# Outputs of the recurrence leave TensorE transposed, with state and values as stationary operands

## The chip, the cores and the metric

The program runs on one core of one Trainium2 chip. The metric is the device time of one execution in microseconds, lower is better. Times of the kernel before are given as the median of three runs; one further execution was recorded by the profiler, and every duration below comes from that one.

## The reference, cut to what matters

Three stages follow each other: a recurrence with one 48x48 state per batch and head (4 batches, 8 heads, 768 time steps), a gated network over 3072 tokens of width 384, and a mixture of eight experts. The change touches the first stage and its hand-over to the second.

```python
B, H, S, D = q.shape                       # 4, 8, 768, 48
k_n = k / (norm(k) + 1e-06)
for t in range(S):
    y[:, :, t] = einsum('bhd,bhde->bhe', q[:, :, t], state)
    v_old = einsum('bhde,bhd->bhe', state, kt)
    state = state + bt * einsum('bhd,bhe->bhde', kt, vt - v_old)
x = y.transpose(0, 2, 1, 3).reshape(B * S, H * D)
gate = 1 / (1 + exp(-(x @ w_gate)))
x = (gate * (x @ w_val)) @ w_out           # then: argmax expert, relu(x @ w1) @ w2, times the gate weight
```

## The kernel before

The program is written by hand, engine by engine, with semaphores; the order in each engine's text is the order in which it works. There is no scheduler.

**Recurrence.** The 768 steps of each batch are cut into chunks of 128 tokens, so there are NG = 24 groups of 128 tokens by 8 heads, worked through batch by batch, chunk after chunk. Two heads make a pair: NPAIR = 4. Inside a group the recurrence becomes a triangular system. A blocked inversion in LEVELS = 7 levels solves it: on each level TensorE forms masked products (L989), VectorE masks them (`level_mask`, L549), TensorE multiplies twice (L997, L1000) and ScalarE copies back (L776, L778). Group g is inverted in step s = g. Group cg = s - 1 is finished in the same step from the inverse found one step earlier: `keys_state` (L956), values W (L1027), `outputs_y` (L1033, L1035), `state_update` (L1043), `y_transposes` (L1049).

**Gated network.** It works on macro tiles of two groups (TB = 256 tokens), LAG = 3 steps behind the recurrence. Its matmuls are cut into 18 pieces a step, `fill(0)` to `fill(17)`, which TensorE's text puts between the pieces of the recurrence: two of three are `products` (nine matmuls, L1062), the third is `project` (six matmuls, L1074). In the first three steps there is nothing to fill with, and `fill` is three throw-away matmuls (`warm`, L1079). The 24 + 3 = 27 steps end near 1000 us; the experts follow.

**How x is made.** TensorE puts the outputs y of a group into PSUM bank pD with tokens on the partitions: for each pair one matmul with the transposed queries as stationary operand and the state as moving operand, 96 columns (L1033), and one for each head with the 128x128 matrix BA as stationary operand and W as moving operand, 48 columns, accumulating (L1035). ScalarE copies pD to `ysb` (L790). Behind `fill(10)` TensorE transposes `ysb` in three 128x128 pieces (L1049) back to pD, since the gated network needs features on the partitions. ScalarE rounds the result to `xh` (L795) and VectorE subtracts to get the low part `xl` (L567); both have the shape 128 x 3 x 256, and `products` reads them as moving operands with the weights' high and low parts.

**pD is one bank with many users in turn:** keys_state, W, y, state update, transposed y, then the transposed keys of the next group. `state_update` waits for `y_ok` (ysb copied), `y_transposes` for `st_ok`, and `key_transposes` and `keys_state` for `xl_ok`.

**Queues around it.** SyncE issues loads in a hand-made order: `load_k`, `load_v`, weight loads in the first three steps, `load_q`. The weights of the gated network pass through two staging buffers; ScalarE rounds them to the high part and GpSimd subtracts to get the low part (L366, L368). TensorE's step 3 begins only when all 18 pieces are done (`wl_ok`).

## Time and profile before

| | |
|---|---|
| Median of three runs | 1403.49 us (1402.86 to 1404.33) |
| The profiled execution's own time | 1403.3 us |
| Its span, first to last instruction | 1401.6 us |
| Mean granted TensorE clock over the span | 0.986 |
| TensorE matmul busy | 1295.3 us, 92% |
| VectorE, ScalarE, GpSimd busy | 41%, 31%, 31% |
| Steps 4 to 23 of the recurrence | 38.4 or 38.5 us each |

The page lists busy time by engine, the span in 40 slices, the chain of work that ended last and the costliest groups of instructions. Matmuls are pipelined: a row of the timeline gives the start of a block, then the time from its first start to its last end, so two blocks overlap in it. What a block takes of TensorE's time is therefore read from the start of one block to the start of the next. A matmul on fp32 data appears as two instructions, one on fp32r or fp16 data, and a transpose, as one.

### The profile page before, as it was taken

The page shows a single profiled execution, that of the slowest core. Times are in us where ns is not written, and L with a number is a line of the kernel's source. Part 1 is how long each engine was busy: PE and PEld are TensorE (multiplying, and loading weights), DVE is VectorE, ACT ScalarE, POOL GpSimd, SP SyncE. Part 2 cuts the span into 40 slices and gives each one's busy share as a digit, 9 for nine tenths or more (in the row PEclk, how much of TensorE's full clock was granted, in tenths as well). Part 3 has the DMA queues.
Part 4 walks back from the last instruction along what each step waited for, and adds up shares of the span by engine and source line. Part 5 has one row for each costly group of instructions (what it writes and reads, how often), then busy time and mean ns, then how long its engine had stood idle before and what let it go on. Part 6 is the DMA issues. An engine that isn't in the chain of part 4 may idle for free.

```text
span 1401.6 us, 28256 instructions
## 1 busy us (share of the span) xinstructions
PE 1295.3 (92%) x11527; PEld 1061.4 (76%) x11527; DVE 578.5 (41%) x1427; ACT 438.2 (31%) x980; POOL 435.7 (31%) x471
## 2 busy tenths in 40 slices
PE   4889999999999999999999999999469999999996
PEld 4567888988888988889888889999435555555553
DVE  1555444555555464645555554533401111111111
ACT  0445334433433434344434333332111111111110
POOL 4565322332333333323323332312222222222210
PEclk9999999999999999999999999999779999999999
DMA  4232000000100000000000000005331333311100
GB/s 138 76 96 63 18 18 30 13 30 19 30 19 25 14 28 18 19 30 13 30 18 30 18 24 13 19 2 192 112 108 52 104 119 121 124 35 34 34 25 1
DMA packets 42796, 66.89 MB, mean 48 GB/s; under 512 B 6345, under 2 KB 34929, under 8 KB 42672
## 3 DMA queue, kind: packets, MB, share of 16 engines
q1 hardware_dynamic: 36944, 54.19, 12.1%
q0 software_dynamic: 5728, 10.91, 2.7%
q8 instruction: 95, 1.56, 0.5%
q14 instruction: 29, 0.24, 0.1%
HBM read 55.29 MB, written 11.16 MB: 47 GB/s over the span
## 4 chain that ended last, share of the span: by engine, by line
PE 82%; DVE 10%; issue 3%; ACT 2%; POOL 1%; DMA 0%; SPq 0%; POOLq 0%; DVEq 0%
PE ps L1062 22%; PE ps L1225 12%; PE ps L1235 11%; PE ps L1074 8%; PE ps L997 3%; PE ps L1027 3%; PE ps L1035 3%; PE ps L1000 2%; DVE BA L540 2%; DVE MP L549 2%; PE ps L972 2%; PE ps L1244 2%; PE ps L1033 2%; PE ps L989 2%; PE ps L956 1%
## 5 line engine op out<-in xcount | busy, mean ns | idle before, releaser
L1062 PE MATMUL ps<-xh,wgh 128*128 128x256 f32 x864 | 265.9, 308 | 0.0
L1062 PE MATMUL ps<-xl,wgh 128*128 128x256 f32 x864 | 243.6, 282 | 0.0
L1062 PE MATMUL ps<-xh,wgl 128*128 128x256 f32 x864 | 243.0, 281 | 0.0
L374 POOL TENSOR_TENSOR gl<-sg,gh 128x256 fp32r<-128x256 f32 x144 | 105.3, 731 | 394.6 <-ACT gh L811 394.6
L1225 PE MATMUL ps<-W,xsT 128*128 x372 | 170.0, 607 | 1.8 <-issue 1.0
L1062 PEld LDWEIGHTS ps<-xh,wgh 128*128 128x128 f32 x864 | 164.0, 190 | 8.1 <-issue 6.9
L1235 PE MATMUL ps<-W,hT 128*128 x496 | 165.1, 486 | 0.9 <-ACT hT L924 0.9
L1062 PEld LDWEIGHTS ps<-xl,wgh 128*128 128x128 f32 x864 | 164.6, 191 | 0.0
L1062 PEld LDWEIGHTS ps<-xh,wgl 128*128 128x128 f32 x864 | 163.8, 190 | 0.0
L572 DVE TENSOR_TENSOR sg<-sg,ps 128x256 f32<-128x256 f32 x144 | 60.5, 420 | 216.5 <-ACT sg L807 216.5
L1235 PEld LDWEIGHTS ps<-W,hT 128*128 128x128 f32 x496 | 94.2, 190 | 73.0 <-issue 15.5
L776 ACT CAST Xs<-ps 128x512 f16<-128x512 f32 x144 | 84.1, 584 | 192.7 <-PE ps L997 192.7
L549 DVE TENSOR_TENSOR MP<-ps,mE 128x512 f16<-128x512 f32 x144 | 98.2, 682 | 101.2 <-PE ps L989 99.6
L1225 PEld LDWEIGHTS ps<-W,xsT 128*128 128x128 f32 x372 | 69.0, 192 | 80.3 <-issue 77.9
L458 POOL DMA_INDIRECT out_dram<-ot,idt x31 | 31.8, 1025 | 283.2 <-DVE ot L748 283.2
L807 ACT ACTIVATE sg<-ps 128x256 f32<-128x256 f32 x144 | 55.3, 384 | 182.5 <-PE ps L1062 182.5
L1074 PE MATMUL ps<-woh,gh 128*128 128x392 f32 x288 | 107.1, 372 | 1.2 <-POOL gl L374 1.2
L1074 PE MATMUL ps<-wol,gh 128*128 128x392 f32 x288 | 98.1, 341 | 0.0
L1074 PE MATMUL ps<-woh,gl 128*128 128x392 f32 x288 | 97.9, 340 | 0.0
L359 POOL TENSOR_TENSOR lof<-CT,BA 128x512 f32<-128x512 f16 x48 | 66.5, 1385 | 80.2 <-DVE CT L543 79.9
L772 ACT CAST Xs<-ps 128x512 f16<-128x512 f32 x48 | 28.1, 585 | 202.6 <-PE ps L979 202.6
L928 ACT COPY xsT<-ps 128x384 f32<-128x384 f32 x31 | 14.8, 479 | 241.9 <-PE ps L1212 218.8
(182 smaller groups left out, 2342.9 us busy)
## 6 DMA issues: line engine op xcount, KB each, us to landing
W<-w_dram SPq DMA_DIRECT2D x16, 1536.0 KB, 11.1
kin<-kv_dram SPq DMA_DIRECT2D x24, 192.0 KB, 2.5
kqT<-qT_dram SPq DMA_DIRECT2D x48, 96.0 KB, 2.5
vin<-kv_dram SPq DMA_DIRECT2D x24, 192.0 KB, 2.4
x_dram<-x2r SPq DMA_DIRECT2D x24, 192.0 KB, 2.0
woT<-woT_dram SPq DMA_DIRECT2D x1, 2304.0 KB, 9.0
stage<-w_gate_dram SPq DMA_DIRECT2D x6, 384.0 KB, 3.2
stage<-w_val_dram SPq DMA_DIRECT2D x6, 384.0 KB, 3.5
```

What stands on the lines that cost most here:

```text
L359: pool.tensor_tensor(lof[:, :, :], CT[:, hs, :], BA[:, 0, hs, :], ALU.add).then_inc(lof_ok, 1)
L374: pool.tensor_tensor(gl[n % 2][:, :], gp[n % 2][:, :], gh[n % 2][:, :].bitcast(F32), ALU.subtract).then_inc(gl_ok, 1)
L549: nc.vector.tensor_tensor(cols(MP[l], l, 0), packed(pC, l), mE[:, l - 1, :].rearrange("p (a c) -> p a c", c=1 << l).unsqueeze(1).to_broadc ...
L572: nc.vector.tensor_tensor(gp[n % 2][:, :], sg[n % 2][:, :], ps[n % 2][:, TB:2 * TB], ALU.mult).then_inc(gp_ok, 1)
L776: nc.scalar.copy(cols(Xs, l, 0), packed(pA, l)).then_inc(xx_ok, 1)
L807: nc.scalar.activation(sg[n % 2][:, :], ps[n % 2][:, 0:TB], ACT.Sigmoid).then_inc(sg_ok, 1)
L997: mm = pe.matmul(packed_head(pA, h, l), XTs[:, h, :], head(MP[l], h, l, 0), start=True, stop=True)
L1027: mm = pe.matmul(pD[:, h * D:(h + 1) * D], XF[:, h, :], Rp[:, h, :], start=True, stop=True)
L1062: mm = pe.matmul(ps[n % 2][:, kind * TB:(kind + 1) * TB], w[:, kind, a, cs], v[m % 2][:, a, :], start=(a == 0 and x == 0), stop=(a == KT - ...
L1074: mm = pe.matmul(ps[2 + j][:, 0:ROW], g[n % 2][:, j * P:(j + 1) * P], w[:, f, :], start=(f == 0 and x == 0), stop=(f == NF - 1 and x == 2))
L1225: mm = pe.matmul(ps[c][:, :], xsT[q][:, a, :], W12[:, bass.ds(s, 1), a * F2 + c * (F2 // 2):a * F2 + (c + 1) * (F2 // 2)].rearrange("p o f ...
L1235: mm = pe.matmul(ps[5 + r][:, 0:HD], hT[r][:, a, :], W12[:, bass.ds(sl, 1), KT * F2 + a * HD:KT * F2 + (a + 1) * HD].rearrange("p o f -> p ...
```

## The change

- **Operands swapped.** In `outputs_y` the state becomes the stationary operand (128 columns: two heads of 48, each padded to 64) and the transposed queries the moving one (128 columns). For each head W becomes stationary (48 columns) and BA moving (128 columns). The result stands in pD with features on the partitions: head 2p on rows 0 to 47, head 2p + 1 on rows 64 to 111, tokens of pair p in columns 128p and on. The state tile is padded for it.
- **Transposes and one copy go.** `y_transposes` with its three matmuls and ScalarE's copy to `ysb` are removed.
- **x is laid out anew.** pD's first three pairs are the three contraction tiles of 128 rows, each with two gaps of 16 rows. The fourth pair goes to a tile `xg`, and six transfers of 16 partitions by 1 KB a group (`spread`, on SyncE's queue) put its rows into the gaps. The rows of the weights are permuted on the host to fit. High and low parts share one tile `xx`.
- **x_high and x_low are two instructions each** (384 and 128 columns) and stand earlier: x_high where ScalarE copied to `ysb`, x_low on VectorE right behind `level_mask(3)`, ahead of the state's update, where it stood behind `level_mask(5)`.
- **Waits.** TensorE's `state_update` waits for `xl_ok` where it waited for `y_ok`. `key_transposes`, `keys_state` and `ranks` wait for `st_ok` where they waited for `xl_ok`. x_high also waits for the transfers of the group before; `products` waits for the transfers of its two groups.
- GpSimd's sum goes into BA in place, where it went into a tile `lof`.

```diff
-    St = sa("St", [P, B, NPAIR, 2 * D])
+    St = sa("St", [P, B, NPAIR, 2, 64])
+    xg = sa("xg", [P, 2, P], F32R)
...
+        def spread(cg):
+            m = cg // 2
+            ts = slice((cg % 2) * P, (cg % 2 + 1) * P)
+            sp.wait_ge(xl_ok, 2 * cg + 2)
+            for a in range(KT):
+                for r in range(2):
+                    sp.dma_start(xx[m % 2][64 * r + D:64 * r + 64, :, a, ts].bitcast(F32), xg[64 * r + 16 * a:64 * r + 16 * a + 16, :, :].bitcast(F32)).then_inc(xg_in, 16)
...
             if s + 1 < NG:
                 load_q(s + 1)
+            if 1 <= s <= NG:
+                spread(s - 1)
             if s < PRE:
                 for n in range(6 * s + 5, min(6 * s + 8, NCW)):
                     load_weights(n)
...
-            pool.tensor_tensor(lof[:, :, :], CT[:, hs, :], BA[:, 0, hs, :], ALU.add).then_inc(lof_ok, 1)
+            pool.tensor_tensor(BA[:, 0, hs, :], CT[:, hs, :], BA[:, 0, hs, :], ALU.add).then_inc(lof_ok, 1)
...
-            wait(dve, xh_ok, cg + 1)
-            nc.vector.tensor_tensor(xl[m % 2][:, :, ts], pD[:, 0:HD].rearrange("p (a t) -> p a t", t=P), xh[m % 2][:, :, ts].bitcast(F32), ALU.subtract).then_inc(xl_ok, 1)
+            wait(dve, xh_ok, 2 * cg + 2)
+            nc.vector.tensor_tensor(xx[m % 2][:, 1, :, ts], pD[:, 0:HD].rearrange("p (a t) -> p a t", t=P), xx[m % 2][:, 0, :, ts].bitcast(F32), ALU.subtract).then_inc(xl_ok, 1)
+            nc.vector.tensor_tensor(xg[:, 1, :], pD[:, HD:], xg[:, 0, :].bitcast(F32), ALU.subtract).then_inc(xl_ok, 1)
...
-            nc.scalar.copy(ysb[:, :, :], pD[:, 0:HD].rearrange("p (h d) -> p h d", d=D)).then_inc(y_ok, 1)
...
+            wait(act, xg_in, 16 * 6 * cg)
+            nc.scalar.copy(xx[m % 2][:, 0, :, (cg % 2) * P:(cg % 2 + 1) * P], pD[:, 0:HD].rearrange("p (a t) -> p a t", t=P)).then_inc(xh_ok, 1)
+            nc.scalar.copy(xg[:, 0, :], pD[:, HD:]).then_inc(xh_ok, 1)
...
-            pe.matmul(pD[:, 2 * p * D:2 * (p + 1) * D], kqT[cg % 2][:, p, 1, :], St[:, cg % B, p, :], start=True, stop=True)
-            for h in (2 * p, 2 * p + 1):
-                mm = pe.matmul(pD[:, h * D:(h + 1) * D], BA[:, 1 + cg % 2, h, :], W[:, h, :], start=False, stop=True, skip_group_check=True)
+            pe.matmul(pD[:, p * P:(p + 1) * P], St[:, cg % B, p, :, :].rearrange("p r c -> p (r c)"), kqT[cg % 2][:, p, 1, :], start=True, stop=True)
+            for r in range(2):
+                mm = pe.matmul(pD[64 * r:64 * r + D, p * P:(p + 1) * P], W[:, 2 * p + r, :], BA[:, 1 + cg % 2, 2 * p + r, :], start=False, stop=True, skip_group_check=True)
...
         def state_update(cg):
-            wait(pe, y_ok, cg + 1)
+            wait(pe, xl_ok, 2 * cg + 2)
...
-            wait(pe, st_ok, cg + 1)
-            for a in range(KT):
-                mm = pe.transpose(pD[:, a * P:(a + 1) * P], ysb[:, :, :].rearrange("p h d -> p (h d)")[:, a * P:(a + 1) * P], mI[:, :])
```

**Place 1: TensorE, the outputs of one pair, between two levels of the inversion.** Names: out<-in, then partitions x columns of the result; ps is PSUM. Before:

```order
L989 MATMUL ps<-Xs,CT 128x64 x7
L1033 MATMUL ps<-St,kqT 128x96 [waits w_ok]
L1035 MATMUL ps<-W,BA 128x48 x2
L1079 MATMUL ps<-mE,mI 128x384 x3
L997 MATMUL ps<-MP,XTs 128x64 [waits mp_ok]
```

The change:

```order
L995 MATMUL ps<-Xs,CT 128x64 x7
L1039 MATMUL ps<-kqT,St 128x128 [waits w_ok]
L1041 MATMUL ps<-BA,W 48x128 x2
L1080 MATMUL ps<-mE,mI 128x384 x3
L1003 MATMUL ps<-MP,XTs 128x64 [waits mp_ok]
```

The place is the same; the operands have changed sides, and the two matmuls with W now write 48 partitions and 128 columns where they wrote 128 partitions and 48 columns.

**Place 2: TensorE, from the state's update to the place of the transposes.** Before:

```order
L1000 MATMUL ps<-XTs,MP 128x64 x8
L1043 MATMUL ps<-W,kb 48x48 [waits y_ok]
L1043 MATMUL ps<-W,kb 48x48 x7
L1079 MATMUL ps<-mE,mI 128x384 x3
L989 MATMUL ps<-Xs,CT 128x64 [waits xx_ok]
L989 MATMUL ps<-Xs,CT 128x64 x7
L1079 MATMUL ps<-mE,mI 128x384 x3
L997 MATMUL ps<-MP,XTs 128x64 [waits xts_ok,mp_ok]
L997 MATMUL ps<-MP,XTs 128x64 x7
L1000 MATMUL ps<-XTs,MP 128x64 x8
L1049 MATMUL ps<-mI,Rp 128x128 [waits st_ok]
L1049 MATMUL ps<-mI,Rp 128x128 x2
```

The change:

```order
L1006 MATMUL ps<-XTs,MP 128x64 x8
L1049 MATMUL ps<-W,kb 48x48 [waits xl_ok]
L1049 MATMUL ps<-W,kb 48x48 x7
L1080 MATMUL ps<-mE,mI 128x384 x3
L995 MATMUL ps<-Xs,CT 128x64 [waits xx_ok]
L995 MATMUL ps<-Xs,CT 128x64 x7
L1080 MATMUL ps<-mE,mI 128x384 x3
L1003 MATMUL ps<-MP,XTs 128x64 [waits xts_ok,mp_ok]
L1003 MATMUL ps<-MP,XTs 128x64 x7
L1006 MATMUL ps<-XTs,MP 128x64 x8
L1080 MATMUL ps<-mE,mI 128x384 x3
```

The transposes are gone, and the update of the state waits for VectorE's x_low. On VectorE the same stretch, from the mask of level 3, was before:

```order
L549 TENSOR_TENSOR MP<-ps,mE 128x64x8 [waits m_ps]
L560 TENSOR_TENSOR St<-St,ps 48x4x48 [waits su_ps]
L560 TENSOR_TENSOR St<-St,ps 48x4x48
L549 TENSOR_TENSOR MP<-ps,mE 128x32x16 [waits m_ps]
L549 TENSOR_TENSOR MP<-ps,mE 128x16x32 [waits m_ps]
L567 TENSOR_TENSOR xl<-ps,xh 128x3x128 [waits xh_ok]
```

and is now:

```order
L558 TENSOR_TENSOR MP<-ps,mE 128x64x8 [waits m_ps]
L576 TENSOR_TENSOR xx<-ps,xx 128x3x128 [waits xh_ok]
L577 TENSOR_TENSOR xg<-ps,xg 128x128
L569 TENSOR_TENSOR St<-St,ps 48x4x48 [waits su_ps]
L569 TENSOR_TENSOR St<-St,ps 48x4x48
L558 TENSOR_TENSOR MP<-ps,mE 128x32x16 [waits m_ps]
```

x_low has moved up by two masks and stands between the mask of level 3 and the state.

**Place 3: SyncE in step 2, around the last weight load.** Before:

```order
L253 DMA stage<-w_out_dram 128x2x384 [waits wl_ok] x3
L243 DMA kqT<-qT_dram 48x4x128 [waits y_ps]
L243 DMA kqT<-qT_dram 48x4x128
L253 DMA stage<-w_out_dram 128x2x384 [waits wl_ok]
L234 DMA kin<-kv_dram 128x384 [waits kn_ok]
```

The change:

```order
L252 DMA stage<-w_out_dram 128x2x384 [waits wl_ok] x3
L242 DMA kqT<-qT_dram 48x4x128 [waits y_ps]
L242 DMA kqT<-qT_dram 48x4x128
L291 DMA xx<-xg 16x2x128 [waits xl_ok]
L291 DMA xx<-xg 16x2x128 x5
L252 DMA stage<-w_out_dram 128x2x384 [waits wl_ok]
L233 DMA kin<-kv_dram 128x384 [waits kn_ok]
```

Six transfers stand ahead of the last weight load.

## Rows read from the trace of the kernel before

**Rows 1.** The page, part 1: busy us, share of the span, instructions.

```profile
PE 1295.3 (92%) x11527; PEld 1061.4 (76%) x11527; DVE 578.5 (41%) x1427; ACT 438.2 (31%) x980; POOL 435.7 (31%) x471
```

**Rows 2.** Waits of TensorE, 160 to 1000 us: total us, times, longest us.

```profile
PE ps L997 <- DVE MP L549: 20.8, 19, 1.1
```

**Rows 3.** Timeline of TensorE, one pair's outputs: start us, us, engine, line, what.

```profile
711.97 0.44 PE L1033 MATMUL ps<-St,kqT 128*128 128x96 f32 x2
712.25 0.57 PE L1035 MATMUL ps<-W,BA 128*128 128x48 f32 x4
712.64 0.36 PE L1062 MATMUL ps<-xh,wgh 128*128 128x256 f32 x1
712.84 0.28 PE L1062 MATMUL ps<-xl,wgh 128*128 128x256 f32 x1
```

**Rows 4.** Timeline of TensorE around the update of the state.

```profile
723.39 0.40 PE L1000 MATMUL ps<-XTs,MP 128*128 128x64 f16 x8
723.72 0.56 PE L1043 MATMUL ps<-W,kb 128*48 128x48 f32 x16
724.21 0.39 PE L1062 MATMUL ps<-xh,wgh 128*128 128x256 f32 x1
724.44 0.28 PE L1062 MATMUL ps<-xl,wgh 128*128 128x256 f32 x1
```

**Rows 5.** Timeline of TensorE around the transposes of y.

```profile
727.03 0.40 PE L1000 MATMUL ps<-XTs,MP 128*128 128x64 f16 x8
727.26 0.52 PE L1049 MATMUL ps<-mI,Rp 128*128 128x128 f32 x3
727.54 0.42 PE L1074 MATMUL ps<-woh,gh 128*128 128x392 f32 x1
```

**Rows 6.** Timeline of TensorE at the step's start, then W.

```profile
701.51 1.03 PE L956 MATMUL ps<-St,kqT 128*128 128x96 f32 x8
702.46 2.00 PE L972 MATMUL ps<-kqT,kbT 48*128 48x256 f32 x16
...
708.65 1.88 PE L1027 MATMUL ps<-Rp,XF 128*128 128x48 f32 x16
710.37 0.39 PE L979 MATMUL ps<-mI,XTs 128*128 128x128 f16 x4
```

**Rows 7.** Timeline of VectorE, same step.

```profile
722.45 0.64 DVE L549 TENSOR_TENSOR MP<-ps,mE 128x512 f16<-128x512 f32 x1
723.01 0.46 DVE L488 TENSOR_SCALAR nsq<-nsq 128x2 f32<-128x2 f32 x1
...
725.84 0.69 DVE L549 TENSOR_TENSOR MP<-ps,mE 128x512 f16<-128x512 f32 x1 [0.72 <-PE ps L989]
...
729.81 0.55 DVE L567 TENSOR_TENSOR xl<-ps,xh 128x384 fp32r<-128x384 f32 x1
```

**Rows 8.** Timeline of VectorE one step earlier, with the choice of experts.

```profile
687.35 0.69 DVE L549 TENSOR_TENSOR MP<-ps,mE 128x512 f16<-128x512 f32 x1 [0.79 <-PE ps L989]
```

**Rows 9.** Timeline of ScalarE, same step as Rows 7.

```profile
719.58 0.50 ACT L790 COPY Rp<-ps 128x384 f32<-128x384 f32 x1
720.68 0.39 ACT L807 ACTIVATE sg<-ps 128x256 f32<-128x256 f32 x1 [0.60 <-PE ps L1062]
```

**Rows 10.** Timeline of SyncE's queue in step 2: start us, us, what.

```profile
116.85 1.21 SPq L243 DMA_DIRECT2D kqT<-qT_dram  x2
119.57 0.37 SPq L253 DMA_DIRECT2D stage<-w_out_dram  x1
```

**Rows 11.** Timeline of TensorE at the start of step 3.

```profile
125.81 1.10 PE L956 MATMUL ps<-St,kqT 128*128 128x96 f32 x8 [1.05 <-POOL wol L368]
```

**Rows 12.** Timeline of GpSimd before the first group.

```profile
12.24 0.83 POOL L348 TENSOR_TENSOR kn<-kin,rn 128x384 f32<-128x384 f32 x1 [1.83 <-DVE rn L510]
```

**Rows 13.** Timeline of step 24: VectorE's row, then TensorE's row.

```profile
944.92 0.42 DVE L572 TENSOR_TENSOR sg<-sg,ps 128x256 f32<-128x256 f32 x1 [4.82 <-ACT sg L807]
...
945.48 0.56 PE L1043 MATMUL ps<-W,kb 128*48 128x48 f32 x16
```

More of the change, by code:

```diff
@@ L666, in body @@
                 level_mask(g, 3)
+            if cg is not None:
+                x_low(cg)
             if settled(s) is not None:
@@ L680, in body @@
                 level_mask(g, 5)
-            if cg is not None:
-                x_low(cg)
             if settled(s) is not None:
@@ L939, in key_transposes @@
             wait(pe, kn_ok, g + 1)
-            wait(pe, xl_ok, g - 1)
+            wait(pe, st_ok, g - 1)
             for p in range(NPAIR):
```

46 lines of the change are left out of this document (19 added, 27 removed).

## The prediction, made before the run

> **What bounds the kernel now.** I read the page's busy times first: TensorE's matmuls are busy 92% of the span, no other engine over 41% [rows 1]. Next TensorE's waits: in the 840 us from 160 to 1000 it waited 20.8 us in 19 stalls of up to 1.1 us for VectorE's masks [rows 2], so nearly everything that is added to or taken from TensorE's row in a step moves the end. Then the timelines, since the blocks' starts tell what each block takes of TensorE. All steps look alike (38.4 us), so I price one and multiply.
>
> **The outputs of a pair, before.** From the first state matmul to the second matmul of the following fill it is 712.84 - 711.97 = 0.87 us: 0.28 for two instructions, 0.39 for four, 0.20 for the first fill matmul [rows 3]. Six full stationary operands are loaded, and that is what it costs: 16 instructions that load 128 fp32 columns and move only 48 take 710.37 - 708.65 = 1.72 us, 0.107 each [rows 6]. So 128 fp32 columns loaded cost 0.107, or 0.84 ns a column, and the 48 or 96 moved columns are hidden behind it. I take the same 0.84 ns for a moved column: three transposes that load 128 and move 128 take 0.28, start included [rows 5].
>
> **The outputs of a pair, after.** State: 128 loaded, 128 moved, twice. W: 48 loaded (0.04), 128 moved (0.107), four instructions, two for each half of the array's columns. Two questions decide.
>
> *Do the halves work at the same time?* The state's update has this shape today: 16 instructions, 48 loaded and 48 moved, alternating between the halves. One after another, at 0.04 each, they would take 0.64; TensorE is at the next block after 724.21 - 723.72 = 0.49 us, everything included [rows 4]. The matmuls on two halves of the rows say the same: 16 of 256 moved columns (0.215 each by 0.84 ns) are through in 2.00 us and not 3.4 [rows 6]. So yes.
>
> *What does it cost to go from the whole array to half arrays and back?* Between blocks of one shape the next starts 0.17 us before the former's last end: 727.26 against 727.03 + 0.40 [rows 5]. Into the state's update it starts only 0.07 before: 723.72 against 723.39 + 0.40 [rows 4]; into the half-row block 0.08 before, 702.46 against 701.51 + 1.03 [rows 6]. So going in costs 0.10. Coming out: the update's last end is 724.28, the fill starts 0.07 before it [rows 4]; in rows 3 it starts 0.18 before (712.64 against 712.82). Another 0.10, and its second matmul comes 0.23 behind the first and not 0.20, since its load is no longer taken ahead. The waits at these blocks are not the reason: the transposes wait for a semaphore too, and start at once.
>
> So a pair takes: the two state instructions 0.28 as now [rows 3], + 0.03 for 32 more moved columns in the first, + 0.10 for the change of shape = 0.41, of which the second's 0.107 is part; the first round of W 0.04 + 0.107 = 0.15; the second round and the way out 0.107 + 0.10 = 0.21; to the fill's second matmul 0.22. Sum 0.99 against 0.87, of which I take 0.98: **+0.11 us a pair, +0.44 a step**. Bounds: with changes of shape of 0.08 and 0.12 it is +0.07 to +0.15 a pair.
>
> The Trainium skill, TensorEngine Tiling, section Tiling Modes (Key Properties), says that changing the tiling mode drains TensorE. The rows above agree, at 0.10 us each way. The same page, section Performance Considerations, recommends just this change, a swap of the operands with column tiling where the moved dimension is 64 or less; by that advice alone a pair would get shorter, and that is my first rival.
>
> **The transposes go:** 727.54 - 727.26 = **-0.28 a step** [rows 5]. ScalarE's copy (0.50) is replaced by a copy of the same 384 columns and one of 128, some 0.3 by the rows of 256 and 384 (0.39, 0.50); pipelined this ends about 0.25 later, and ScalarE was idle for 0.60 before its next sigmoid [rows 9]. Cost nothing. If that cover were gone, the sigmoid, VectorE's product and the mask of level 3 would be late by the rest.
>
> **The new wait.** The mask of level 3 ends at 723.09 and the next instruction starts at 723.01 [rows 7]. x_low's first part takes 0.55 [rows 7]; the second, a third of the columns, I take at 0.28, its floor being rows of 0.16 for tiny ones and its ceiling the first's 0.55. Both overlap by 0.08: done at 723.76, or 724.03 by the ceiling. TensorE starts about 0.06 later, at 723.82, where it now starts at 723.72 [rows 4]: **+0.10 a step**, bounds 0 and 0.37. Behind that wait stand on TensorE the update, fill(9) and all that follows. On VectorE the state's addition, the root or the choice of experts move back by 0.67; before the mask of level 4 there are 0.72 and 0.79 us of idle time in the two kinds of steps [rows 7, 8], just enough. x_low's old place frees VectorE where nobody waits.
>
> Steps 3 to 23, 21 of them: 0.44 - 0.28 + 0.10 = +0.26 each, **+5.5 us**. The stalls for masks do not absorb it: they run from the end of a fill through ScalarE and VectorE to the next product, and the pair's outputs stand ahead of that fill.
>
> **Step 24** has no inversion. VectorE's product ends at 945.34 [rows 13], x_low would be done at 946.1, TensorE would start its update at 946.15 and not 945.48: +0.67 + 0.44 - 0.28 = **+0.8 us**.
>
> **Steps 1 and 2** have only throw-away fills; the place of the transposes is partly given back to the wait for ScalarE: about +0.3 each, **+0.6**.
>
> **SyncE's queue.** In step 2 the queue ends load_q at 118.06 and issues the last weight load at 119.57 [rows 10]. Six transfers now stand between. An issue takes 0.37 for that load and 0.60 for half of load_q; with 32 short pieces I take the small end: 6 x 0.37 = 2.2, so 120.3, **+0.75 us** for the start of step 3, since TensorE already waits 1.05 there for the last low part [rows 11]. Bounds: 0.5, and 6 x 0.60 for +2.1. In later steps the queue holds back only load_k by 2.2 us, needed half a step later. The transfers leave by 726 us in the step of rows 7; `products` reads them at the earliest in the next step, after 701.51 + 38.4 = 740, so a landing of up to 14 us is hidden.
>
> **At nothing:** the clearing of the larger state tile (GpSimd waits 1.83 for VectorE after it [rows 12]), GpSimd's sum in place, the permuted weights, the waits that move from xl_ok to st_ok, both of which are then done long before (TensorE's large waits are those for masks [rows 2]).
>
> **Sum:** 5.5 + 0.8 + 0.6 + 0.75 = +7.7 us on the profiled execution's 1403.3 (span 1401.6 and 1.7 around it), 1411.0. The median lies 0.2 above that execution; I leave it at 1411.0. From the bounds: low 4 x 0.07 - 0.28 + 0 = 0 a step, +2 us in all, 1405; high 0.60 - 0.28 + 0.37 = 0.69 a step, 14.5 + 1.5 + 1.3 + 2.1 = +19.5, 1423.
>
> **Rivals.**
>
> *No drain between state and W matmuls* (the change does what it says). The loads for the half arrays are taken ahead as between equal shapes. Then a pair is 0.19 + 0.11 + 0.11 + 0.11 + 0.20 = 0.72, 0.15 less than now. A step: -0.60 - 0.28 + 0.10 = -0.78; 21 of them -16.4, step 24 -0.2, steps 1 and 2 -1.3, the queue +0.75: -17, **1386**. For it: these state and W matmuls follow without a wait, while both half-array blocks of today begin behind a semaphore. Against it: the way out is slow in rows 4 too, and other blocks behind waits are not. The rule on mode switching in the Trainium skill, TensorEngine Tiling, is against it. It decides if a change of shape costs under 0.05 us.
>
> *Halves one after another.* With 128 moved columns from four different tiles the two halves could serialise: +0.215 a pair, +0.86 a step, +20.6 over 24 steps, **1432**. Against it both kinds of half-array blocks [rows 4, 6].
>
> *The drain is partly hidden,* or x_low's wait is nil: the low bound and below, 1390 to 1404. It could be if only the way in or only the way out costs 0.10: -0.4 a step against my sum, -9.6 over 24 steps, **1401**.
>
> *x_low late.* If ScalarE's two copies or VectorE's subtractions take 0.5 longer together, the update waits for them each step: +10 us, **1421**, within my range.
>
> **How the numbers follow.** My forecast, 1405 to 1419: 0.62. x_low late, 1419 to 1424: 0.08. Serial halves, 1425 and over: 0.06. Partly hidden drain, 1390 to 1405: 0.12. No drain, about 1386: 0.12. The range 1401 to 1424 holds the first two and most of the fourth, about 0.8. A measurement can tell 0.2% or 2.8 us from no change: faster is below 1400.7, no drain and a third of the partly hidden, 0.16; the same is 0.11; slower is 0.73.
>
> **What would show it.** In the changed kernel's timeline a pair should take 0.98 us from the first state matmul to the second fill matmul, with the W block starting no earlier than 0.1 us before the state block's last end, and W's four instructions in two rounds 0.15 apart. The update should start 0.6 to 0.7 us behind the second product block of level 3. Steps 4 to 23 should last 38.7 us. Step 3 should start 2 us later than at 125.81, with its part from six issues of about 0.37 us. I am wrong if a pair takes under 0.87, and by how much tells which rival it was.

## The result: 1.1% slower, twice as much as forecast

| | median | range | runs |
|---|---|---|---|
| before | 1403.47 us | 1402.86 to 1404.33 | 4 |
| the change | 1419.27 us | 1418.64 to 1419.74 | 4 |

The ratio is 1.0112, with a 95% interval from 1.0094 to 1.0129: +15.8 us, where +7.7 was forecast. The profiled execution's span is 1417.4 us (1401.6 before), its mean granted clock 0.982 (0.986 before).

The page of the changed kernel, part 1 (busy us, share, instructions), answers to [rows 1]: TensorE has 72 instructions fewer (24 groups of three transposes) and is busy 10.3 us longer.

```profile
PE 1305.6 (92%) x11455; PEld 1038.6 (73%) x11455; DVE 581.0 (41%) x1451; ACT 433.6 (31%) x980; POOL 436.5 (31%) x471
```

I first asked where in the program the time was lost. The start of `keys_state` (L956 before, L962 now) marks each step:

| start of | before | after | lost in the step ahead of it |
|---|---|---|---|
| step 1 | 66.51 | 66.93 | 0.4 |
| step 2 | 95.57 | 96.15 | 0.2 |
| step 3 | 125.81 | 131.11 | **4.7** |
| step 4 | 163.41 | 172.09 | **3.4** |
| step 24 | 930.35 | 943.98 | 4.95 in 20 steps |
| last instruction | 1401.6 | 1417.4 | 2.2 |

More than half is lost in steps 2 and 3, for which I had forecast 1.3 us. The 20 steps from 4 to 23 lose 0.25 each on average, where I had said 0.26: nineteen of them lose 0.20 to 0.24 and step 12 loses 0.65, which the experiments below explain. (Step 23 is shorter than the others in both kernels, 36.74 us before and 36.96 now.) Of the last 2.2, 0.65 lies in the rest of the recurrence; 0.9 is a longer wait for a transfer at the start of the experts (14.9 for 14.0). That wait lay between 13.0 and 15.1 in the traces of this case, and both ends were measured in kernels without the new outputs, so it is scatter and no effect of the change. The last 0.6 lies in the experts and is unexplained.

**The start.** Step 1 begins 0.4 us late. GpSimd clears the larger state tile in 1.80 us where it took 1.37, and the VectorE instruction on 8 columns that started meanwhile lasts until that is done; GpSimd then waits for VectorE's result. First before, then now (start us, us, engine, line, what):

```profile
8.53 1.37 POOL L385 MEMSET St<- 128x1536 f32 x1
9.28 0.65 DVE L488 TENSOR_SCALAR n<-n 128x8 f32<-128x8 f32 x1
```

```profile
8.55 1.80 POOL L394 MEMSET St<- 128x2048 f32 x1
9.30 1.07 DVE L497 TENSOR_SCALAR n<-n 128x8 f32<-128x8 f32 x1
```

**Steps 1 and 2, the queue.** SyncE's queue in the changed kernel (start us, us, what), first in step 1, then in step 2:

```profile
89.58 4.54 SPq L291 DMA_DIRECT2D xx<-xg  x6
94.16 0.58 SPq L252 DMA_DIRECT2D stage<-w_val_dram  x1
...
119.46 1.25 SPq L242 DMA_DIRECT2D kqT<-qT_dram  x2
120.75 3.81 SPq L291 DMA_DIRECT2D xx<-xg  x6
124.60 0.58 SPq L252 DMA_DIRECT2D stage<-w_out_dram  x1
```

The six transfers hold the queue for 3.81 and 4.54 us, 0.6 each (one of them 1.3), and not 2.2. The weight load behind them in step 1 stood at 90.49 before. The last weight load in step 2 is issued at 124.60, 5.0 us later than in [rows 10]. Who waits for these loads: ScalarE in both steps, in step 2 GpSimd behind it, and TensorE behind each of them.

```profile
97.57 0.83 ACT L808 CAST wgh<-stage 128x768 fp32r<-128x768 f32 x1 [3.52 <-DMA stage<-w_val_dram]
98.30 1.07 ACT L792 COPY XF<-ps 128x512 f32<-128x512 f32 x2
```

```profile
99.03 1.53 PE L978 MATMUL ps<-kqT,kbT 48*128 48x256 f32 x11 [1.85 <-ACT XF L792]
```

```profile
129.07 1.82 POOL L377 TENSOR_TENSOR wol<-stage,woh 128x768 fp32r<-128x768 f32 x1 [4.02 <-ACT woh L811]
```

In step 1 ScalarE stands in front of the late weight; behind it in its own row is the copy of XF, which has nothing to do with weights, and TensorE waits 1.85 us for that. So step 2's queue starts late already: load_q ends at 120.71 (119.46 + 1.25) and not at 118.06.

**Step 3, the clock.** TensorE at the start of step 3, answering to [rows 11]:

```profile
131.11 1.99 PE L962 MATMUL ps<-St,kqT 128*128 128x96 f32 x8 [3.90 <-POOL wol L377]
133.03 3.79 PE L978 MATMUL ps<-kqT,kbT 48*128 48x256 f32 x16
```

It waits 3.90 us where it waited 1.05, and then the first block takes 1.99 us where it took 1.10. The view by windows (us, busy us and instructions of five engines, granted clock, DMA share, GB/s) says why:

```profile
126.00:130.00 4.00, 1.21 (x14) 0.66 (x11) 0.04 (x1) 1.83 (x4) 0.93 (x1) 0.93 0.46 144
130.00:134.00 4.00, 2.89 (x12) 2.63 (x14) 1.39 (x2) 0.14 (x1) 1.69 (x2) 0.50 0.00 0
134.00:138.00 4.00, 4.00 (x20) 2.95 (x17) 2.72 (x5) 0.00 (x0) 0.70 (x1) 0.50 0.18 49
138.00:142.00 4.00, 4.00 (x32) 3.91 (x31) 3.00 (x5) 2.25 (x3) 3.28 (x3) 0.79 0.00 0
142.00:146.00 4.00, 4.00 (x46) 3.61 (x46) 1.00 (x2) 1.27 (x3) 1.90 (x2) 1.00 0.01 4
```

The row's engines are TensorE, its weight loads, VectorE, ScalarE and GpSimd. The granted clock begins to fall during the wait (0.93 in its window), is 0.50 (1.2 GHz) behind it and comes back to 1.00 (2.4 GHz) within the window from 138 to 142. Before, it was 1.00 in all windows from 122 to 142. Step 3 is 3.4 us longer; the third experiment shows that 3.1 of them are the clock.

**A step behind that.** One pair's outputs (timeline of TensorE), answering to [rows 3]:

```profile
724.23 0.47 PE L1039 MATMUL ps<-kqT,St 128*128 128x128 f32 x2
724.62 0.42 PE L1041 MATMUL ps<-BA,W 128*48 128x128 f32 x4
724.98 0.50 PE L1063 MATMUL ps<-xx,wgh 128*128 128x256 f32 x2
725.32 0.27 PE L1063 MATMUL ps<-xx,wgl 128*128 128x256 f32 x1
```

From the first state matmul to the fill it is 0.75 us (0.67 before). The W block starts 0.08 before the state block's last end (724.62 against 724.70), and the fill 0.06 before W's last end, though nothing here waits for a semaphore. Going on to the third fill matmul takes 0.34 where a fill elsewhere in this kernel takes 0.32. In all a pair takes 0.97 against 0.87; 0.98 was forecast.

The update, answering to [rows 4], and VectorE ahead of it, answering to [rows 7]:

```profile
736.06 0.40 PE L1006 MATMUL ps<-XTs,MP 128*128 128x64 f16 x8
736.47 0.56 PE L1049 MATMUL ps<-W,kb 128*48 128x48 f32 x16
```

```profile
735.12 0.64 DVE L558 TENSOR_TENSOR MP<-ps,mE 128x512 f16<-128x512 f32 x1
735.67 0.55 DVE L576 TENSOR_TENSOR xx<-ps,xx 128x384 fp32r<-128x384 f32 x1
736.14 0.28 DVE L577 TENSOR_TENSOR xg<-ps,xg 128x128 fp32r<-128x128 f32 x1
```

x_low ends at 736.42 and the update starts at 736.47, 0.41 behind the start of the product block ahead of it; before it was 0.33 [rows 4]. The wait costs about 0.09 a step.

### The profile page after: what moved, and what is told of

Its sections match the earlier page's. It is cut to its first block, busy times and chain, and to the rows that moved or that the text cites. A ratio compares the mean times of both kernels' runs of the same rounds, so it can differ in the third digit from the quotient of the medians.

```text
span 1417.4 us, 28313 instructions
## 1 busy us (share of the span) xinstructions
PE 1305.6 (92%) x11455; PEld 1038.6 (73%) x11455; DVE 581.0 (41%) x1451; ACT 433.6 (31%) x980; POOL 436.5 (31%) x471
## 4 chain that ended last, share of the span: by engine, by line
PE 82%; DVE 9%; issue 4%; ACT 2%; POOL 2%; DMA 1%; SPq 0%; POOLq 0%; DVEq 0%; ACTq 0%
PE ps L1063 23%; PE ps L1224 12%; PE ps L1234 11%; PE ps L1075 8%; PE ps L1033 3%; PE ps L1003 3%; PE ps L978 3%; PE ps L1041 2%; PE ps L1006 2%; DVE MP L558 2%; PE ps L1039 2%; PE ps L1243 2%; PE ps L995 2%; PE ps L962 1%; DVE BA L549 1%
## 5 line engine op out<-in xcount | busy, mean ns | idle before, releaser
L1063 PE MATMUL ps<-xx,wgh 128*128 128x256 f32 x1728 | 345.0, 296 | 0.0
L1063 PEld LDWEIGHTS ps<-xx,wgh 128*128 128x128 f32 x1728 | 266.3, 190 | 20.7 <-issue 19.5
L1063 PE MATMUL ps<-xx,wgl 128*128 128x256 f32 x864 | 243.1, 281 | 0.0
L1063 PEld LDWEIGHTS ps<-xx,wgl 128*128 128x128 f32 x864 | 164.3, 190 | 0.0
L467 POOL DMA_INDIRECT out_dram<-ot,idt x31 | 31.8, 1024 | 283.8 <-DVE ot L758 283.8
L368 POOL TENSOR_TENSOR BA<-CT,BA 128x512 f32<-128x512 f16 x48 | 66.5, 1385 | 80.6 <-DVE CT L552 80.2
L934 ACT COPY xsT<-ps 128x384 f32<-128x384 f32 x31 | 14.9, 479 | 243.0 <-PE ps L1211 218.9
L752 DVE TENSOR_SCALAR hs_<-ps 128x512 f32<-128x512 f32 x31 | 21.4, 692 | 163.8 <-PE ps L1224 163.8
L1003 PE MATMUL ps<-MP,XTs 128*128 128x64 f16 x1152 | 59.2, 195 | 31.8 <-DVE MP L558 28.9
```

Of the source, the lines that this page charges most:

```text
L368: pool.tensor_tensor(BA[:, 0, hs, :], CT[:, hs, :], BA[:, 0, hs, :], ALU.add).then_inc(lof_ok, 1)
L1003: mm = pe.matmul(packed_head(pA, h, l), XTs[:, h, :], head(MP[l], h, l, 0), start=True, stop=True)
L1063: mm = pe.matmul(ps[n % 2][:, kind * TB:(kind + 1) * TB], w[:, kind, a, cs], xx[m % 2][:, v, a, :], start=(a == 0 and x == 0), stop=(a == ...
```

## The experiments

Times are compared with the kernel before on the same chip: 1403.04 us (9 runs) for the first four, 1404.05 (15 runs) for the fifth, 1403.34 (9 runs) for the two kernels of the sixth. Five runs of one kernel spread over 3 to 4 us, so a difference of two medians is good to about 2 us; undisturbed steps of one kind agree within 0.1 in a trace. My theory at this point: of the 15.8 us some 7 are the costs in every step that I had forecast, and the rest comes from six transfers that stand ahead of two weight loads: late loads, and the clock behind the wait.

**Transfers behind the weight loads.** In SyncE's text the two blocks change places:

```diff
-            if 1 <= s <= NG:
-                spread(s - 1)
             if s < PRE:
                 for n in range(6 * s + 5, min(6 * s + 8, NCW)):
                     load_weights(n)
+            if 1 <= s <= NG:
+                spread(s - 1)
```

> The changed kernel with one edit: in steps 1 and 2 the six transfers stand behind the weight loads on SyncE's queue, not ahead of them. Theory A (the queue): the changed kernel's step 2 began 0.6 us late, but lasted 34.96 us and not 30.23, and step 3 40.98 and not 37.61, because the weight loads behind the transfers left 3.7 and 5.0 us later than before, and TensorE's wait of 3.9 us then dropped its clock. With the order turned round the two steps should last 30.4 and 37.9, the clock stay at 1.0 from 60 us on, and the time be 1419.3 - 8.1 = 1411.2 (1410 to 1412.5). Theory B (the early steps are long because of the new outputs and waits themselves): nothing moves, 1419.

Measured: 1410.38 us (1409.41 to 1412.85), ratio 1.0052 [1.0039, 1.0066]: +7.3 us. SyncE's queue in step 2, then TensorE at step 3:

```profile
119.84 0.37 SPq L252 DMA_DIRECT2D stage<-w_out_dram  x1
120.26 3.82 SPq L291 DMA_DIRECT2D xx<-xg  x6
```

```profile
126.12 1.10 PE L962 MATMUL ps<-St,kqT 128*128 128x96 f32 x8 [1.01 <-POOL wol L377]
```

The load is back at 119.84 and the wait at 1.01, the clock stays at 1.00, step 2 lasts 30.20 us, where it lasted 34.96, and step 3 lasts 37.86, where it lasted 40.98. The other steps are what they were, 38.60 and 38.73. So 8.5 of the 15.8 us come from where the six transfers stand (by the traces 4.8 + 3.1, and 0.2 in step 1).

**The kernel before, with six transfers in steps 1 and 2.** Nothing of the change but throw-away transfers of the same shape between two tiles (and GpSimd's sum in place, to make room):

```diff
             if s + 1 < NG:
                 load_q(s + 1)
+            if 1 <= s < PRE:
+                sp.wait_ge(dm_ok, 1)
+                for a in range(KT):
+                    for r in range(2):
+                        sp.dma_start(dmy[64 * r + D:64 * r + 64, :, a, :], dmx[64 * r + 16 * a:64 * r + 16 * a + 16, :, :]).then_inc(dm_in, 16)
             if s < PRE:
```

> The kernel before, plus in steps 1 and 2 only six transfers of 16 partitions by 1 KB from one unused tile to another, at the place on SyncE's queue where the change has them; GpSimd's sum is in place, as in the change, to make room. Outputs, transposes and waits are those of before. Theory A: the cost of the first steps comes with the transfers alone: 1403.5 + 8 = 1411.5 (1410 to 1413), each issue takes 0.6 us, step 2 is 4 to 5 us longer and step 3 about 3. Theory B: 1403.5, no change.

Measured: 1412.11 us (1410.76 to 1413.69), ratio 1.0061 [1.0048, 1.0075]: +9.1 us. Waits of TensorE from 90 to 160 us (total, times, longest), and a window of step 3 and one of step 2:

```profile
PE ps L966 <- POOL wol L377: 4.4, 1, 4.4
...
PE ps L982 <- ACT XF L792: 2.6, 1, 2.6
```

```profile
136.00:140.00 4.00, 4.00 (x20) 2.91 (x17) 2.41 (x6) 0.00 (x0) 0.30 (x1) 0.50 0.17 49
```

```profile
100.00:104.00 4.00, 4.00 (x19) 2.41 (x15) 2.46 (x5) 0.00 (x0) 1.79 (x3) 0.50 0.52 170
```

The transfers alone, in a kernel without the new outputs, do the same damage, by the same two waits. Here the shorter wait is 2.6 us and not 1.85, and the clock fell behind it too: in the profiled execution step 2 is 7.5 us longer and step 3 3.8, more than the 4 to 5 and 3 that I had expected. That execution is the slowest of the five (1413.69, mean clock 0.980); the fastest had 0.985, so the clock need not fall so far each time.

**TensorE kept busy while it waits.** The changed kernel with 20 throw-away matmuls at the end of step 2, so that the loads are as late as before but TensorE doesn't stand still:

```diff
             fill(17)
+            if s == LAG - 1:
+                warm(20)
```

> The changed kernel with 20 more throw-away matmuls of 384 fp16 columns (0.16 us each, 3.3 us) at the end of step 2, inside TensorE's wait of 3.9 us for the last weight piece. The wait on the semaphore stays, step 3 begins at the same time. Theory A1 (half of the loss is the clock): the granted clock stays at 1.0 through 129 to 140 us, step 3 lasts 37.9 and not 41.0 us, the time is 1419.3 - 3.1 = 1416.2 (1415.5 to 1417). Theory A2 (step 3 is long for another reason, such as late transfers or ScalarE): 1419.3, step 3 stays at 41.

Measured: 1415.29 us (1413.92 to 1417.08), ratio 1.0089 [1.0075, 1.0103]: +12.3 us. TensorE's start of step 3 and the clock there:

```profile
131.95 1.10 PE L962 MATMUL ps<-St,kqT 128*128 128x96 f32 x8 [0.46 <-POOL wol L377]
```

```profile
134.00:138.00 4.00, 3.48 (x32) 2.91 (x28) 3.68 (x7) 0.74 (x2) 1.60 (x2) 1.00 0.17 49
```

The loads come as late as in the changed kernel (step 2 lasts 35.10 us for 34.96; step 1 began 0.9 later in this trace, as in two others, for which no edit gives a reason), but step 3 starts at the full clock and lasts 37.86 us. The time is 0.2 us below the range that I had given. The 15.8 us now come apart, by medians: 7.3 for all that is not the queue (the first experiment), 4.9 for the late loads (12.3 - 7.3), 3.5 for the clock (15.8 - 12.3). The traces say 4.8 for the loads (step 2, 34.96 for 30.20) and 3.1 for the clock (step 3, 40.98 for 37.86).

**The values in one block.** This tests the price of changing the array's shape. Without a change of shape in every pair there should be two changes in a step for the outputs and not eight. The first experiment's kernel, with the state's matmuls where they were and all W matmuls behind the last of them:

```diff
-            pe.matmul(pD[:, p * P:(p + 1) * P], St[...], kqT[...], start=True, stop=True)
-            for r in range(2):
-                mm = pe.matmul(pD[64 * r:64 * r + D, p * P:(p + 1) * P], W[:, 2 * p + r, :], BA[...], start=False, stop=True, skip_group_check=True)
+            pe.matmul(pD[:, p * P:(p + 1) * P], St[...], kqT[...], start=(p == 0), stop=True, skip_group_check=True)
+            if p == NPAIR - 1:
+                for q in range(NPAIR):
+                    for r in range(2):
+                        mm = pe.matmul(pD[64 * r:64 * r + D, q * P:(q + 1) * P], W[:, 2 * q + r, :], BA[...], start=False, stop=True, skip_group_check=True)
```

> e1 with another order on TensorE: the state matmul of each pair stays where it is, all eight matmuls with W follow in one block behind the fourth pair's. The half-array block is entered and left once a step and not four times. Theory C (a change of shape costs 0.10 us each way): a state block alone costs 0.50 from its first start to the second fill matmul, three of them 1.50; the last with the W block 0.31 + 0.10 + 0.04 + 8 x 0.107 + 0.10 + 0.21 = 1.62; 3.12 a step against 4 x 0.98 = 3.92, so 0.8 less a step, steps of 37.9 us, and 1411.2 - 19 = 1392 (1389 to 1395). Theory D (the cost lies in the moved columns, not in the change of shape): all columns are still moved, steps stay at 38.7 and the time at 1411.

Measured: 1394.37 us (1392.49 to 1395.81), ratio 0.9935 [0.9921, 0.9948]: 8.7 us faster than the kernel before. The first pair and the last (timeline of TensorE):

```profile
705.08 0.47 PE L1039 MATMUL ps<-kqT,St 128*128 128x128 f32 x2
705.30 0.48 PE L1064 MATMUL ps<-xx,wgh 128*128 128x256 f32 x2
...
710.45 0.47 PE L1039 MATMUL ps<-kqT,St 128*128 128x128 f32 x2
710.84 1.08 PE L1043 MATMUL ps<-BA,W 128*48 128x128 f32 x16
711.85 0.50 PE L1064 MATMUL ps<-xx,wgh 128*128 128x256 f32 x2
```

A state block alone costs 0.22, and the fill follows it 0.25 before its last end: no change of shape, no gap. The W block's 16 instructions take 1.01. That makes 3 x 0.22 + 1.40 = 2.06 us of outputs in a step, where the changed kernel has 4 x 0.75 = 3.00. Steps of 38.73 us became 37.73, which is 1.00 for three entries and three exits fewer: 0.33 for an entry and an exit together. I had reckoned 0.20. By the unrounded starts of the single instructions, the way in costs 0.09 (0.395 from the state block to W, 0.301 without a change of shape), the first round of W 0.04 more than a later one, and the way out 0.17: the fill starts 0.20 behind the last half-array matmul, and 0.03 behind the last whole-array one. The rest is 0.02 at the fill's second matmul.

Two things took part of the gain back: from step 8 on every second step became 38.05 and not 37.6, and steps 1 and 2 became 1.1 and 0.9 longer than in the first experiment. Both are taken up below.

**The values' operand padded to the whole array.** The same price in another way, with the order of the change left as it is: W is padded with zeros to 128 columns a head, so no instruction of a pair has another shape.

```diff
-    W = sa("W", [P, H, D])
+    W = sa("W", [P, NPAIR, 3, 64])
...
-                mm = pe.matmul(pD[64 * r:64 * r + D, p * P:(p + 1) * P], W[:, 2 * p + r, :], BA[...], ...)
+                mm = pe.matmul(pD[:, p * P:(p + 1) * P], W[:, p, r:r + 2, :].rearrange("p a d -> p (a d)"), BA[...], ...)
```

> The kernel of e1_transfers_last with one change: W is padded with zeros, so that for each head the stationary operand of the values' outputs is 128 columns wide (the other head's 64 columns are zero) and writes all 128 rows of pD. No instruction of a pair's outputs changes the shape of the array any more; results are the same. More columns are loaded (128 for 48) and the two heads of a pair can no longer run side by side. What remains of a half-array shape in a step is the update of the state and the half-row block, as in the kernel before. My theory (the change of shape costs 0.10 us each way): the W block starts some 0.17 us before the state block's last end, a pair takes 0.19 + 4 x 0.11 + 0.11 + 0.20 = 0.94 us where e1 takes 0.98, steps 4 to 23 last 38.5 us where e1's last 38.6 to 38.7, 1407 us (1405.5 to 1409). Rival (the wait ahead of W is not for the shape but for accumulating onto columns that the state's matmul has just written): the W block still starts 0.02 us or less before the state block's last end, a pair takes 1.05 us or more, steps 39.0, about 1418 us. Second rival (the halves did not run side by side at all, so nothing is lost by padding and the wait stays): 1410, as e1.

Measured: 1404.65 us (1403.32 to 1406.63, 11 runs), ratio 1.0008 [0.9999, 1.0017]. That is below the range that I had given. The pair:

```profile
712.67 0.47 PE L1040 MATMUL ps<-kqT,St 128*128 128x128 f32 x2
712.98 0.61 PE L1042 MATMUL ps<-BA,W 128*128 128x128 f32 x4
713.34 0.48 PE L1064 MATMUL ps<-xx,wgh 128*128 128x256 f32 x2
```

The W block starts 0.16 before the state block's last end, and accumulates onto columns that it has just written: so the gap is for the shape, not for the accumulation. Four passes and the way to the fill take 0.36, just as the half-array version takes in two rounds with two changes of shape. What is gained is the way in: 0.31 for 0.39. With 0.20 to the second fill matmul a pair is 0.87 us, the price of the kernel before; I had expected 0.94, having counted the last pass whole, although the fill starts 0.03 behind its start. Steps of the odd kind last 38.30, 0.43 less than in the first experiment, four times 0.11. A start 1.4 us later takes part of it back: 0.7 because GpSimd clears W ahead of its first keys, and 0.7 between 45 and 51 us, unexplained. And four of its even steps last 38.62 and not 38.19.

**Where the steps of 38.05 come from.** In the kernel with the values in one block TensorE waits once more in these steps, and VectorE's row ahead of that has no idle time. VectorE and GpSimd in such a step, then the same two instructions in step 6 of the same trace, which lasts 37.62:

```profile
722.86 0.41 PE L1003 MATMUL ps<-MP,XTs 128*128 128x64 f16 x8 [0.27 <-DVE MP L558]
```

```profile
721.33 0.73 POOL L383 TENSOR_TENSOR gl<-sg,gh 128x256 fp32r<-128x256 f32 x1 [2.22 <-ACT gh L819]
721.34 0.74 DVE L504 SCALAR_TENSOR_TENSOR nx<-nx 128x2 f32<-128x2 f32 x1
722.11 0.69 DVE L558 TENSOR_TENSOR MP<-ps,mE 128x512 f16<-128x512 f32 x1
```

```profile
267.06 0.77 POOL L383 TENSOR_TENSOR gl<-sg,gh 128x256 fp32r<-128x256 f32 x1 [2.22 <-ACT gh L819]
267.06 0.16 DVE L504 SCALAR_TENSOR_TENSOR nx<-nx 128x2 f32<-128x2 f32 x1
```

L504 is the last of the six instructions of a square root on two columns, right ahead of the mask. It takes 0.16 us or 0.74. When it takes 0.74, it started 5 to 11 ns behind GpSimd's product and ends 0.02 us behind that product's end; when it takes 0.16 there, it started 1 to 6 ns behind it. Which of the two happens is thus a matter of a few ns. I had expected only that the six instructions fill the row (they take 1.1 us undisturbed) and that TensorE now comes too early; but all 18 steps that are 0.43 too long have this long L504, and no other step from 4 to 23 has it: 8 steps here, 5 in a second run of this kernel, 4 in the padded kernel, and step 12 of the changed kernel, whose row on TensorE is not shorter but longer. So a shorter row is not needed for it. In the kernel before, GpSimd's product starts 0.2 us behind the end of the root and VectorE has 0.33 of idle time ahead of that mask; in the changed kernel the two meet and the idle time is 0.06.

I moved three of the six instructions behind the mask, and ran the kernel without that beside it:

```diff
         def gate_b(m):
             root_step(nsq[:, 2 * m:2 * m + 2], nx[:, 3, :], nx[:, 4, :], nx[:, 5, :])
-            root_step(nsq[:, 2 * m:2 * m + 2], nx[:, 3, :], nx[:, 4, :], nx[:, 5, :])
 
         def gate_c(m):
+            root_step(nsq[:, 2 * m:2 * m + 2], nx[:, 3, :], nx[:, 4, :], nx[:, 5, :])
```

> The kernel of e5_values_in_one_block with one change on VectorE: of the two root steps between the mask of level 4 and the mask of level 5 (six instructions on a few columns, in every second step), the second (three instructions, about 1.2 us with the waits between them) moves behind the mask of level 5. In e5 the steps without these instructions last 37.7 us, 1.00 less than in e1, as its shorter outputs say; the steps with them last 38.05, only 0.56 less, with a new wait of 0.27 us of TensorE for the mask of level 5 (instruction L1003), which VectorE starts without any idle time before it. My theory (TensorE now arrives before VectorE has got through its small instructions, so in these steps part of the gain is given back): the wait of 0.27 goes, all steps from 6 on last 37.6 to 37.7, total -0.4 x 9 = -3.6 us against e5 on the same chip, 1390.5 to 1391.5 us. Rival (the mask is late for its own input, and VectorE's small instructions only fill the time): no change against e5, 1394. Second rival (the moved instructions delay VectorE's product of the gate or the mask of level 6 instead): the wait of 0.27 moves to the next level, 1393 to 1396.

> The kernel of e5_values_in_one_block once more, so that e8_root_split has it beside it on the same chip: 1394.4 us as before, 1393 to 1396, with steps of 37.7 and 38.05 us.

Measured: 1391.06 us (1389.29 to 1393.32), ratio 0.9912 [0.9898, 0.9925], with the root split, and 1391.80 (1391.24 to 1395.04), ratio 0.9922 [0.9908, 0.9935], without. Waits of TensorE from 160 to 920 us, first with the split, then without:

```profile
PE ps L1003 <- DVE MP L558: 20.8, 19, 1.1
```

```profile
PE ps L1003 <- DVE MP L558: 22.1, 24, 1.1
```

With the split no step is longer than 37.74 and the sum of these waits is again what it was before the change [rows 2]; L504 no longer meets GpSimd's product. The split removes the long steps, as forecast. Its size is not 3.6 us: in the run beside it the long L504 came only in five steps of ten, and steps 4 to 23 together are 2.2 us shorter with the split. The two medians differ by 0.7, less than the runs scatter; the same kernel gave 1394.37 in the first series and 1391.80 here, below the 1393 that I had expected. That 1391.06 fell into its forecast range is luck.

Steps 1 and 2 show the same meeting and one thing more. Without the split they are 0.9 to 1.1 us longer than in the first experiment: two VectorE instructions on 8 columns (L503, L517) take 1.55 and 1.67 us, each until GpSimd's subtraction for a weight is done, and TensorE waits 1.75 for the mask behind them. With the split they are longer by another 1.0 and 0.6, and that is the clock. The window from 86 to 90 us, first with the split, then without:

```profile
86.00:90.00 4.00, 3.98 (x58) 2.67 (x55) 1.64 (x5) 2.35 (x5) 2.04 (x2) 0.65 0.27 88
```

```profile
86.00:90.00 4.00, 3.68 (x70) 2.39 (x66) 1.66 (x5) 2.87 (x6) 2.02 (x2) 1.00 0.26 90
```

The wait ahead of it is 1.75 us in both.

**What an issue costs.** Two kernels with throw-away transfers on SyncE's queue in the middle of the kernel, where nobody waits for the queue. They differ from the second experiment in the shapes:

```diff
+            if s == 5:
+                sp.wait_ge(dm_ok, 1)
+                for a in range(KT):
+                    sp.dma_start(dmy[:, 0, a, :], dmx[:, 0, :]).then_inc(dm_in, 16)
...
+            if s == 11:
+                for a in range(KT):
+                    sp.dma_start(dmy[0:16, 0, a, :], dmx[0:16, 0, :]).then_inc(dm_in, 16)
```

> The kernel before, with GpSimd's sum in place, no transfers in steps 1 and 2, and on SyncE's queue three throw-away transfers between tiles in SBUF in each of six later steps, ahead of nothing that is urgent, each with another shape: step 5 with 128 partitions x 512 B, step 7 with 128 partitions x 2 pieces of 512 B, step 9 with 64 partitions x 2, step 11 with 16 partitions x 1 from partition 0, step 13 with 16 partitions x 2 from partition 0, step 15 with 16 partitions x 2 to partitions 48 and on. It measures how long one issue holds the queue. My prediction took 0.37 us for a transfer of 16 partitions, from a weight load of 128 partitions; the changed kernel shows 0.60 to 0.64. Theory A (an issue is dear where the partitions are fewer than 128): 0.33 to 0.40 in steps 5 and 7, 0.6 in the other four. Theory B (it is dear where a partition has two pieces): 0.6 in steps 7, 9, 13, 15 and 0.35 in steps 5 and 11. Theory C (transfers from SBUF to SBUF are dear whatever their shape): 0.6 in all six. The time should be that of the kernel before, 1403.5 +- 2.

```diff
+            if s == 9:
+                for a in range(2):
+                    sp.dma_start(dmy[:, a, 0:P], kv_d[0, :, 0:P]).then_inc(dm_in, 16)
```

> As e6_issue_times_by_shape, which showed 0.59 to 0.68 us for all six shapes of transfers between tiles in SBUF, 128 partitions x 512 B included. Left open: load_q reads from DRAM and takes 0.57 to 0.60 too, so the source alone may not be the reason; weight and token loads (0.33 to 0.38) have pieces of 1536 or 3072 B. Two throw-away transfers in each of six steps: step 5 SBUF to SBUF, 128 partitions x 1024 B; step 7 SBUF to SBUF, 16 partitions x 1024 B; step 9 DRAM to SBUF, 128 x 512 B; step 11 DRAM to SBUF, 16 x 512 B; step 13 DRAM to SBUF, 128 x 2 pieces of 512 B; step 15 DRAM to SBUF, 16 x 2 pieces of 512 B. Theory C (a source in SBUF makes it dear, something else makes load_q dear): 0.6 in steps 5 and 7, 0.33 to 0.43 in steps 9 to 15. Theory D (pieces of 512 B are dear): 0.35 in steps 5 and 7, 0.6 in the other four. Theory E (the second and later of several issues in a row behind load_q is dear, whatever it moves): 0.6 in all. The time should be that of the kernel before, 1403.5 +- 2.

Measured: 1403.2 and 1404.1 us, one run each, beside 1404.05 (15 runs) and 1404.93 (one run) of the kernel before. The queue in the first kernel with 128 and with 16 partitions, then in the second with 128 partitions from DRAM:

```profile
221.15 1.89 SPq L304 DMA_DIRECT2D dmy<-dmx  x3
...
451.85 1.87 SPq L313 DMA_DIRECT2D dmy<-dmx  x3
```

```profile
375.06 1.07 SPq L310 DMA_DIRECT2D dmy<-kv_dram  x2
```

Between tiles of SBUF an issue holds the queue for 0.58 to 0.68 us with 16, 64 or 128 partitions, one piece or two, 512 or 1024 B (one of 22 took 1.18). From DRAM the first of two took 0.59 and the second 0.42 to 0.47, again whatever its shape. So it was not the 32 short pieces: the shape doesn't matter, and theories A, B, D and E fall. C holds only in part. In these traces a load from DRAM right behind load_q or behind a transfer from SBUF took 0.58 to 0.60, whatever it was; behind another load it mostly took 0.43 or 0.47. Why that is so, and why load_q takes 0.6 and kin's load after a pause 0.34, stays open.

## Why the prediction went wrong, step by step

**The step that failed is the queue, and in it four things.** I wrote +0.75 us with a bound of 2.1; it is 8.5.

- *The price of an issue.* I took "the small end", 0.37 from a weight load. [Rows 10] offered 0.60 from half of load_q as well, and about 0.6 it was: 3.8 us for six and not 2.2 (4.5 in step 1, where one took 1.3). With the large end alone the last load would have been 2.1 late.
- *The place.* Six transfers are issued in step 1 as well, ahead of a weight load, and I priced the queue in step 2 only. The load was 3.7 us late there (94.16 for 90.49). I had not asked who stands behind it on ScalarE: a copy on TensorE's path, worth 1.85 us of waiting, and the delay went on into step 2's queue. 2.65 us carried over (0.5 of them also without the queue's part: load_q ends at 118.59 in the first experiment), plus 3.9 for the six, less the 1.5 of slack that [rows 10] show, is the 5.0 us that the last load is late.
- *The end of the chain.* TensorE already waited for the last low part [rows 11], so there was no slack on its side, and all of it arrives: 131.11 for 125.81.
- *The clock.* I did not think of it. A wait that grows from 1.05 to 3.90 us took the clock to its lower level for the blocks behind it, and that cost another 3.1 us by the traces, 3.5 by the medians.

**What held, and what only seemed to.** Without the queue my sum was 6.9 us (5.5 + 0.8 + 0.6); the kernel with the transfers out of the way measures +7.3. That the two are so close is in part luck. Steps 3 to 23 gave 4.9 and not 5.5, and steps 1 and 2 nothing (29.03 and 30.20 for 29.07 and 30.23) where I had 0.6. Against that stand two things that I had not: 0.4 at the start, which I had put at nothing (I asked only whether GpSimd waits behind the clearing, and not whether VectorE is held by it), and 0.7 outside the span (2.4 us around it for 1.7), which no row explains. Steps: 38.7 forecast, 38.60 and 38.73 measured. The wait of the update: +0.10 forecast, 0.09 measured. The transposes: three matmuls of 0.28 together are gone. Step 24 and what is left of the recurrence: 0.8 forecast, 0.65 measured.

A pair of outputs: 0.98 forecast, 0.97 measured, but not by 0.10 for each change of shape. The way in costs 0.09 and the way out 0.17. My way out of 0.10 stood behind a last round that I had counted whole, although a fill starts 0.03 behind the start of the last matmul where the shape stays. For the pair the two errors cancel; for the values in one block they do not, and there the outputs became 1.00 us shorter a step (0.94 up to the fills' starts) and not 0.80.

Two of my signs did not follow from my own sum. The update starts 0.41 behind the second product block (my sum says 0.43; the 0.6 to 0.7 that I wrote holds from the first product block), and my sum for the start of step 3 was 1.35 late and not 2. It was 5.3.

**The rivals.** No drain (1386) and serial halves (1432) both fall at the pair: 0.97. The partly hidden drain falls there too. x_low late (1419 to 1424) takes in the measured 1419.27, but its mechanism is not what happened: the update waits 0.09 and not 0.6. That the time lies within my range of 1401 to 1424 is luck as well, since 8.5 of the 15.8 us come from the queue, which I had at 0.75. Halves do work side by side: the W block's 16 instructions take 1.01 us, 0.06 each, where a whole-array instruction of the same length takes 0.11. That the stalls for masks don't absorb a longer row was right (21.0 us in 20 stalls for 20.8 in 19, the one more being step 12's). What I had not asked is what VectorE's row, moved by x_low and by the missing transposes, would meet on GpSimd: I looked at the idle time before the mask of level 4 and not before that of level 5.

**Changing the shape.** The Trainium skill, TensorEngine Tiling (Array Packing), section Tiling Modes (Key Properties), says that changing the tiling mode drains TensorE. The traces here agree, with 0.33 us for a way in and out. The Trainium skill, TensorEngine Tiling (Array Packing), section Performance Considerations, recommends the swap with column tiling for a moved dimension of 64 or less. By this case that holds if the blocks of one shape are long enough: spread over the pairs it cost 0.11 us a pair, in one block it made the kernel 0.7 to 0.8% faster.

## What to carry to other kernels

A swap to half-array operands pays by block, not by instruction: gather all matmuls of that shape into one block before counting its gain. A few small transfers cost a queue their issue time, so take the dearest row that the trace has for one, list every load behind them in every stage (the start-up above all, where the queue is the bound), and ask who stands behind the engine that waits. Where a wait of TensorE grows by some us, price the blocks behind it at the lower clock as well; and when a change moves VectorE's row, look at what GpSimd does at the new time: an instruction of a few columns that starts just behind a long one there can last as long as that.

## What the runs showed of the hardware

- Changing from whole-array to half-array fp32 matmuls and back costs TensorE 0.33 us, with no semaphore between them: 0.09 going in (state to W 0.30 without the change, 0.39 with it), 0.04 in the first round, 0.17 coming out (the fill starts 0.20 behind the last half-array matmul, 0.03 behind the last whole-array one) and 0.02 behind that. In this kernel, a stretch of 0.36 us holds either two rounds on halves with the way out, or four passes on the whole array.
- After TensorE stood still for 3.90 us its granted clock was 0.50 for the blocks behind it, which took 1.99 and 3.79 us where they take 1.10 and 2.00, and was 1.00 again from 142 us on. It fell after waits of 2.6 and 4.4 us too. After waits of 1.01, 1.05 and 1.85 us it stayed at 1.00. After waits of 1.74 to 1.77 us it fell in one trace (twice) and stayed at 1.00 in two traces of the same work on TensorE (twice each). With throw-away matmuls in the wait it stayed at 1.00.
- A VectorE instruction of a few columns can last as long as a GpSimd instruction beside it. In the eleven traces, up to 1000 us, 324 VectorE instructions with a result of 2 or 8 columns took over 0.6 us (undisturbed 0.16 to 0.25), and 320 of them ended within 0.1 us of the end of a GpSimd instruction that had started ahead of them. All of these were TENSOR_SCALAR or SCALAR_TENSOR_TENSOR; reciprocals of that size took their usual 0.2 beside GpSimd's work.
- Behind the six transfers from SBUF the next load holds the queue for 0.58 us, where a weight load otherwise takes 0.33 to 0.38 after a pause and 0.43 behind another, so they slow one more issue than their own.
